# Last 64 tokens' keys and values of batches 1 to 3: two heads side by side in 64 partitions, or one above the other in 128

## The reference

```
kv  = einsum('bhsd,bhse->bhde', k, v)       # 4 batches, 8 heads, 576 tokens, head size 64
out = einsum('bhsd,bhde->bhse', q, kv)
out = out / sqrt(mean(out * out, -1) + 1e-6) * g_norm
x   = out.transpose(0, 2, 1, 3).reshape(2304, 512)
x   = (silu(x @ w_gate) * (x @ w_val)) @ w_out        # hidden size 1536
x   = softplus(x @ w_in2) @ w_out2                    # hidden size 2048
```

## Time and profile before

| | |
|---|---|
| median of three runs | 886.56 us (886.12 to 887.71) |
| the profiled execution's own time | 886.71 us |
| span of its instructions | 884.9 us |
| TensorE matmuls busy | 876.9 us, 99% of the span |
| mean granted TensorE clock over the span | 0.998 |
| VectorE, ScalarE, GpSimd busy | 73%, 50%, 26% |
| moved by DMA | 53.93 MB in 95541 packets |
| matmuls of `kv_product` (line 905) on the chain that ended last | 1.1% of the span |

### The profile page before, as it was taken

How to read it: one execution, slowest core, us unless ns; L and a number is a source line. 1 busy time by engine, 2 the same in 40 slices (tenths; PEclk the granted TensorE clock), 3 DMA queues, 4 the chain that set the end, 5 groups by cost and what they waited for, 6 DMA issues and landing times.

```text
span 884.9 us, 14699 instructions
## 1 busy us (share of the span) xinstructions
PE 876.9 (99%) x5362; PEld 814.6 (92%) x5362; DVE 649.9 (73%) x1254; ACT 440.5 (50%) x778; POOL 230.0 (26%) x189
## 2 busy tenths in 40 slices
PE   8999999999999999999999999999999999999998
PEld 7999999999999999999999998998998999999997
DVE  3655655788585877676777998878878878878875
ACT  4627454765342534342445764544554554554553
POOL 4643203599511399630255000000000000000000
PEclk9999999999999999999999999999999999999999
DMA  9985765542100022100033110000000000000100
GB/s 274 221 209 155 158 132 134 153 128 73 37 1 1 1 72 73 46 16 1 1 118 122 48 48 0 36 0 0 36 0 0 36 0 0 36 0 0 37 1 36
DMA packets 95541, 53.93 MB, mean 61 GB/s; under 512 B 37248, under 2 KB 86528, under 8 KB 95488
## 3 DMA queue, kind: packets, MB, share of 16 engines
q1 hardware_dynamic: 95328, 53.23, 22.3%
q10 hardware_dynamic: 160, 0.00, 0.0%
HBM read 44.96 MB, written 8.26 MB: 60 GB/s over the span
## 4 chain that ended last, share of the span: by engine, by line
PE 97%; DMA 1%; issue 1%; SPq 1%; ACT 0%; DVE 0%; POOL 0%; DVEq 0%; POOLq 0%
PE bank L972 23%; PE bank L974 23%; PE bank L973 23%; PE bank L1131 8%; PE bank L1130 7%; PE bank L1129 7%; PE bank L912 1%; PE bank L905 1%; PE bank L980 1%; PE bank L878 0%; PE bank L986 0%; DMA v_rest<-in_v 0%; PE bank L867 0%; DMA q<-in_q 0%; SPq L502 0%
## 5 line engine op out<-in xcount | busy, mean ns | idle before, releaser
L972 PE MATMUL bank<-x_hi,arena 128*128 128x384 f32 x554 | 187.0, 338 | 0.0
L974 PE MATMUL bank<-x_hi,arena 128*128 128x384 f32 x554 | 186.8, 337 | 0.0
L973 PE MATMUL bank<-x_lo,arena 128*128 128x384 f32 x554 | 186.0, 336 | 0.0
L972 PE MATMUL bank<-ring,slots 128*128 128x256 f32 x504 | 142.7, 283 | 0.3 <-DVE sum_b L1616 0.3
L974 PE MATMUL bank<-ring,slots 128*128 128x256 f32 x504 | 142.6, 283 | 0.0
L973 PE MATMUL bank<-ring,slots 128*128 128x256 f32 x504 | 142.6, 283 | 0.0
L1354 ACT ACTIVATE act_a<-bank 128x384 f32<-128x384 f32 x96 | 47.2, 492 | 173.9 <-PE bank L974 173.9
L1131 PE MATMUL bank<-arena,g_lo 128*128 128x512 f32 x288 | 113.1, 393 | 0.0
L1130 PE MATMUL bank<-arena,g_hi 128*128 128x512 f32 x288 | 112.9, 392 | 0.0
L1129 PE MATMUL bank<-arena,g_hi 128*128 128x512 f32 x288 | 111.9, 388 | 0.0
L972 PEld LDWEIGHTS bank<-x_hi,arena 128*128 128x128 f32 x554 | 104.4, 188 | 4.0
(11 more groups left out here) (140 smaller groups left out, 1657.5 us busy)
## 6 DMA issues: line engine op xcount, KB each, us to landing
stage<-in_moe_w_out SPq DMA_DIRECT2D x28, 256.0 KB, 3.5
out_dram<-out_stage SPq DMA_DIRECT2D x18, 256.0 KB, 2.1
k<-in_k SPq DMA_DIRECT2D x16, 256.0 KB, 3.3
v<-in_v SPq DMA_DIRECT2D x16, 256.0 KB, 3.3
stage<-in_moe_w_in SPq DMA_DIRECT2D x16, 256.0 KB, 2.8
xy<-in_q SPq DMA_DIRECT2D x48, 72.0 KB, 3.0
stage<-in_moe_w_gate SPq DMA_DIRECT2D x12, 256.0 KB, 3.7
stage<-in_moe_w_val SPq DMA_DIRECT2D x12, 256.0 KB, 4.1
```

Source lines behind the costliest of these rows:

```text
L972: nc.tensor.matmul(ps, hi, rhs_hi, start=first, stop=False)
L973: nc.tensor.matmul(ps, hi, rhs_lo, start=False, stop=False)
L974: return nc.tensor.matmul(ps, lo, rhs_hi, start=False, stop=last)
```

## The change

`k_rest` and `v_rest` of batches 1 to 3 become tiles of 128 partitions and 64 elements. The even head's 64 tokens lie in partitions 0 to 63, the odd head's in 64 to 127. The DMA's source is now written `heads[:, KROWS:S, :]`, head first and token second, where it was token first and head second; number, order and semaphores of the DMAs stay. It still moves 128 runs of 256 bytes. The rest products take their operands from partitions `odd * D` to `odd * D + 63`, so the odd head's reads the upper half. A new tile `pairs_rest` that nothing uses keeps all later tiles at their addresses. The attention of batch 0 is left as it is.

```diff
     def pair_buffers(n):
         return {"k": sb(f"k{n}", [P, 2, J, D], F32), "v": sb(f"v{n}", [P, 2, J, D], F32),
-                "k_rest": sb(f"k_rest{n}", [REST, 2, D], F32), "v_rest": sb(f"v_rest{n}", [REST, 2, D], F32)}
+                "k_rest": sb(f"k_rest{n}", [P, D], F32), "v_rest": sb(f"v_rest{n}", [P, D], F32)}
 
     pairs = [pair_buffers(f"_{n}") for n in range(2)]
+
+    sb("pairs_rest", [P, 4 * D], F32)
...
-                sp.dma_start(to[n + "_rest"][:, :, :],
-                             heads[:, KROWS:S, :].rearrange("h p d -> p h d")).then_inc(loaded, 16)
+                sp.dma_start(to[n + "_rest"][:, :], heads[:, KROWS:S, :]).then_inc(loaded, 16)
...
             for j in range(NT):
                 for odd in range(2):
-                    l, r = [bufs[x][:, odd, j, :] if j < J else bufs[x + "_rest"][:, odd, :] for x in "kv"]
+                    l, r = [bufs[x][:, odd, j, :] if j < J else bufs[x + "_rest"][odd * D:(odd + 1) * D, :] for x in "kv"]
```

## The result

| | before | after |
|---|---|---|
| median of 13 runs | 886.56 us (886.03 to 888.46) | 889.34 us (887.69 to 890.15) |
| ratio | | 1.0024, 95% interval 1.0016 to 1.0033 |
| profiled execution's own time | 886.71 us | 889.59 us |

The change costs 0.24%, some 2.1 us. The ratio is that of the means; the medians stand 2.78 us apart and the profiled executions 2.88. The lines of the page on the packets come first, of the kernel before and then of the kernel after, because they show what the transfers did.

The account below looks back on a forecast made before the run. The prediction took TensorE's queue as the bound, matmuls busy 99% of the span. It summed 886.71 + 1.8 for the wait + 0 for the products = 888.5 us, 888.4 against the median, range 886.2 to 890.6.

Parts of the forecast that it names:

- The share-out of the transfer: Rest transfers with 2 heads outermost would occupy only 2 DMA engines, 64 packets each in place of 8.
- The price of a packet: A 256-byte packet was put at 20 ns at most, so a rest transfer costs each of two engines 1.28 us.
- The wait ahead of pair (3,3): Last v_rest would land at 153.3 us, not 151.44, so TensorE starts that pair 1.8 us later (1.5 to 2.6).
- the same sum: Lower end for the last v_rest landing: 143.75 + 1.2 + 4 x (0.83 + 1.28) = 153.4 us, less 0.5 over-counting.
- SyncE's issue: 0.61 us per rest transfer, may change with the pattern; decides nothing with two engines, could win 0.45 us with 16.
- The rest products: Twelve pairs of 4 matmul records on TensorE's path: taken as 0, bounds 1.3 us gained or 1.3 us lost.
- The other pairs: Pairs ahead of the last two have room: (2,2), (2,3) issued 8 us before use, delay at most 4.5 us; no wait.
- step 3's weights: Queued behind (1,0) and (1,1), last part 4.5 us later; low part done at 39.2 us, wanted at 39.85: hidden by 0.6.
- this rival: Step 3's weights come too late, before 39.85 us, if a packet costs over 23 ns; 892.6 us at 30 ns; chance 0.05.
- The clock: Rival: idle of 2.3 us ahead of pair (3,3) also drops the granted clock, 1.7 us more, 890.1 us; chance 0.25.
- The row that the prediction went by: Before the change, TensorE idled 1.19 us before 9.01 us; granted clock of the next 4 us was 0.57.
- the delay is added to the time in full: Whatever delays the last v_rest landing, ahead of pair (3,3), lengthens the whole time by as much: 1.8 us.

## Why the prediction was right, and what it missed

It said 888.4 us, in a range of 886.2 to 890.6, and more likely slower than the same. Measured: 889.34. By the ratio, 2.1 us with 1.4 to 2.9 as its ends, against the 1.8 that it summed. The mechanism was the right one, but that the total fits so well is in part luck: one term was too large (1.8 us for a wait of 1.29) and one was missing (1.24 us).

*The share-out of the transfer: right.* The packets show two engines. The rule of the Trainium skill on the number of engines ("DMA: Bandwidth & Descriptors", why a DMA increments its semaphore by 16) agrees with this row: 14 semaphore writes fewer for each transfer. That this is what matters is shown by the pair of runs with the extra copies, 907.88 against 890.51 us.

*The price of a packet: too high.* The sum took 20 ns, from the busy share of a stretch with all engines at work. In the kernel after, the stretch from 146.8 to 147.1 us has only two engines at rest packets:

```profile
DMA packets 60, 0.03 MB, mean 97 GB/s; under 512 B 42, under 2 KB 60, under 8 KB 60
```

42 of 256 bytes and 18 of 1 KB are 29.2 KB, which is 97 GB/s x 0.3 us, so the 42 are all rest packets. Two engines do 42 in 0.3 us, 14 ns each, which is 0.91 us for 64, not 1.28. The packet records have 18 ns for the length of each, so packets overlap on an engine, and busy time per packet is not the distance from one to the next.

*The wait ahead of pair (3,3): mechanism right, 1.29 us more instead of 1.8.* With the right price the same sum, 143.75 + 1.2 + 4 x (0.83 + 0.91), ends at 151.9, and the landing, with the 0.36 us taken off, was at 152.7. The packets of the four rests show where the other 0.8 us went (start of the first, start of the last; us, in the kernel after):

| rest transfer | first packet | last packet |
|---|---|---|
| `k_rest` (3,2) | 146.44 | 147.34 |
| `v_rest` (3,2) | 148.42 | 149.54 |
| `k_rest` (3,3) | 150.02 | 151.13 |
| `v_rest` (3,3) | 151.61 | 152.73 |

The first one starts 0.3 us later than reckoned. From one rest to the next it is 1.98, then 1.60 and 1.59 us, where the sum has 1.74. The last one takes 1.12 us, because one of its two engines runs 0.23 us behind the other, and it has landed 0.36 us behind its last packet; the sum had 0.91 for both.

SyncE's issue stalls as well: 1.39 us for the `v` of pair (3,3) in place of 0.59, so that the last `v_rest` was issued 5.07 us behind the first `k`, not 4.35.

```profile
144.11 0.45 SPq L505 DMA_DIRECT2D k<-in_k  x1
...
147.75 1.39 SPq L505 DMA_DIRECT2D v<-in_v  x1
149.18 0.53 SPq L507 DMA_DIRECT2D v_rest<-in_v  x1
```

That stall is not what makes the landing late. In all five profiles with changed last pairs and no copies (the changed kernel, only the last two pairs, and the three with moved loads) the last three rests start 1.59 to 1.61 us apart on their engines, while SyncE issues them 1.16 to 2.00 us apart. The two engines set the pace. "With two engines behind, it decides nothing", the prediction said of SyncE's issue, and there it held.

*The rest products: 0, as taken.* In pair (1,0) the four rest records still take 0.27 us, start to next start, against 0.26. Neither the gain of up to 1.3 us that a weight load beside the other half's product would bring, nor the loss of as much from two row tiles in one bank, is seen:

```profile
50.27 0.33 PE L907 MATMUL bank<-v_rest,k_rest 64*64 64x64 f32 x4
50.54 0.44 PE L974 MATMUL bank<-x_hi,arena 128*128 128x384 f32 x1
```

*The other pairs, and step 3's weights: hidden, as said.* The run with all but the last two pairs changed costs nothing. Here SyncE's stalls show: the last part of step 3's weights was issued at 27.30 us, where it was 24.91 before.

```profile
27.30 0.84 SPq L577 DMA_DIRECT2D stage<-in_moe_w_out  x1
...
31.54 1.49 ACT L1240 ACTIVATE arena<-stage 128x1536 fp32r<-128x1536 f32 x1 [1.16 <-DMA stage<-in_moe_w_out]
```

Its rounding started at 31.54 us, 1.6 us later than before, of which 0.36 is the start; 4.5 was reckoned. At 14 ns a packet the same reckoning gives 4 x 56 x 14 ns = 3.1, so the price explains only a part. GpSimd's low parts of steps 2 and 3 end at 36.66 us, with 3.5 us to spare and not 0.6. That is 36.29 and the shift of 0.36, so nothing was lost: GpSimd has step 2's part to do until 33.0 us, which is when the rounding ended. The prediction put the low part behind the late rounding without looking at what GpSimd does meanwhile, and started from an issue time that could itself move. In the run with copies of 2 heads outermost this rival came true, 2.2 us at that place.

*The clock: not in the kernel after, but in a run beside it.* From 154.1 to 158 us after, the granted clock was 1.00. In the run with copies of 64 tokens outermost, a wait of 2.47 us was followed by 0.57, its lower level for 3.4 us of four; the run with one transfer per head waited 2.49 us and kept 1.00. The prediction had it decide from about 1.2 us; here 1.74 us did nothing, and at about 2.5 us it went either way. The row that the prediction went by, is no firmer: the profile with only the last two pairs changed has an idle of 0.95 us there, as the changed kernel has 0.96, and its clock from 9 to 13 us is 1.00 where the changed kernel's is 0.57. No run shows what decides it. The stretch behind the wait of 2.47 us:

```profile
154.00:158.00 4.00, 4.00 (x19) 4.00 (x17) 1.37 (x4) 0.00 (x0) 0.00 (x0) 0.57 0.56 169
```

*What was missed:* the 1.24 us between 204 and 213 us. The prediction wrote that the delay is added to the time in full, "since no other engine's lateness stands beside it". But the delay did not move all engines alike: SyncE's next load had a condition of its own. The sum with nothing added would have held only if everything behind had moved by the same amount. The runs on it show the mechanism in their profiles: the same idle with old tiles and an earlier load, none with new tiles and a later one.

Two things stay open. The subtraction behind the cast takes 1.53 us in one case and 0.98 or 0.99 in the other, which is half of VectorE's 1.1 us, and no run takes it apart. And the intervals of the small ratios overlap, so that the split of 2.1 us into the wait and the later idle rests on one profile of each kernel and not on the times.

## What to carry to other kernels

Read a DMA's two patterns from the outside in: a reshape that puts 2 heads ahead of 64 tokens leaves the bytes, the packets of data and the destination's 128 partitions alone and takes 14 of 16 engines away. The count of small packets on the page of the profile shows it at once. Such a transfer may be harmless in ten places and cost its whole delay in the eleventh, so look for the one load that TensorE already waits for, and where nothing else helps, issue that one earlier. And when a delay enters a tuned schedule, ask which engines do not move with it: a meeting of VectorE and GpSimd that was decided by 0.07 us may come out the other way fifty microseconds later.

## What the runs showed that I had not expected

- Where transfers pile up, SyncE's issue of the next one takes longer, also when that one needs all sixteen engines: 1.82 us for one issue at 19.31 and at 21.78 us after, where the longest of the same eight issues took 1.21 before. It is not peculiar to a backlog on two engines: in the run with one transfer per head, where every rest has sixteen, one issue of step 2's weights, ahead of all those rests, took 2.46 us. The DMA engines' busy share from 17 to 21 us was 1.18 there. What the limit is, no run shows.

```profile
17.24 2.46 SPq L578 DMA_DIRECT2D stage<-in_moe_w_out  x1
```

- Packets of 256 bytes follow each other every 14 ns on an engine that has only them, though each is 18 ns long in the packet records.
- Whether a VectorE cast starts 0.07 us ahead of a GpSimd operation or 0.01 us behind it decides 0.58 us of the cast, and 1.24 us of TensorE in the steps that follow.
